# Constant products on TensorE, masks by halves, maxima by tiles and a later weight load in a kernel of clustered attention and two MLPs

## The reference, cut to what is computed

```python
# q, k, v: (2, 8, 768, 64); centroids: (8, 16, 64)
q_assign = argmax(einsum('bhsd,hcd->bhsc', normed(q), normed(centroids)), axis=-1)
k_assign = argmax(einsum('bhsd,hcd->bhsc', normed(k), normed(centroids)), axis=-1)
mask = q_assign[:, :, :, None] == k_assign[:, :, None, :]
scores = where(mask, scale * q @ k.T, -1e9)
attn = exp(scores - max(scores)); attn = attn / (sum(attn) + 1e-9)
x = (attn @ v) as (1536, 512)
# twice: h = x @ w_in (512 -> 2048); g = f(h); x = g @ w_out (2048 -> 512)
# first f: relu with a slope per unit; second f: a ratio of a cubic and a square of h
```

## Time and profile before

| what | us |
|---|---|
| median of 3 runs | 801.58 |
| lowest and highest of them | 801.36 and 802.98 |
| profiled execution, its own time | 800.81 |
| its span | 798.9 |
| TensorE busy (matmuls) in it | 783.6 |
| VectorE busy | 556.3 |
| ScalarE busy | 491.0 |
| GpSimd busy | 295.2 |

### The profile page before, as it was taken

One profiled execution on the slowest core, in us unless ns is written; L12 is line 12 of the kernel. 1 busy time (PEld: TensorE's weight loads), 2 busy tenths in 40 slices (PEclk: granted clock), 3 DMA queues, 4 the chain that ended last, 5 costly groups with the idle time before them and its releaser, 6 DMA issues.

```text
span 798.9 us, 13162 instructions
## 1 busy us (share of the span) xinstructions
PE 783.6 (98%) x4345; PEld 740.3 (93%) x4345; DVE 556.3 (70%) x963; ACT 491.0 (61%) x857; POOL 295.2 (37%) x330
## 2 busy tenths in 40 slices
PE   6999999999999999999999999999999999999997
PEld 5988999999999999999999999999988998999896
DVE  5678878878875555444444454478888888888886
ACT  3766777777887111211211144389999999999996
POOL 7777888988983896000000046540000000000000
PEclk9999999999999999999999999999999999999999
DMA  7636474474332332000000035410001001001001
GB/s 195 187 104 140 119 190 129 118 195 128 83 103 74 100 106 80 0 0 0 0 0 0 0 86 152 123 37 1 1 1 39 0 0 39 0 0 39 1 1 39
DMA packets 30310, 52.15 MB, mean 65 GB/s; under 512 B 9181, under 2 KB 11322, under 8 KB 30266
## 3 DMA queue, kind: packets, MB, share of 16 engines
q1 hardware_dynamic: 30266, 51.59, 23.3%
HBM read 29.40 MB, written 3.19 MB: 41 GB/s over the span
## 4 chain that ended last, share of the span: by engine, by line
PE 83%; DVE 8%; ACT 6%; issue 1%; SPq 1%; DMA 1%; ACTq 0%; DVEq 0%
PE ps L207 28%; PE ps L1193 16%; PE ps L1204 12%; PE ps L724 4%; PE ps L757 4%; PE ps L770 4%; PE ps L809 4%; PE ps L801 4%; PE ps L802 4%; PE ps L694 2%; DVE g_f L1355 1%; ACT scratch L1271 1%; DVE corr L1342 1%; DVE scratch L1351 1%; ACT scratch L1269 1%
## 5 line engine op out<-in xcount | busy, mean ns | idle before, releaser
L213 ACT ACTIVATE g_hi<-g_f 128x384 fp32r<-128x384 f32 x128 | 67.3, 526 | 215.7 <-PE ps L1193 192.5
L217 DVE TENSOR_TENSOR g_lo<-g_f,g_hi 128x384 fp32r<-128x384 f32 x128 | 78.8, 615 | 82.9 <-ACT g_hi L213 82.9
L207 PE MATMUL ps<-x_hi,w_hi_b 128*128 (+1 forms) x352 | 118.8, 337 | 0.0
L207 PE MATMUL ps<-x_hi,w_lo_b 128*128 (+1 forms) x352 | 118.7, 337 | 0.0
L207 PE MATMUL ps<-x_lo,w_hi_b 128*128 (+1 forms) x352 | 118.7, 337 | 0.0
L930 ACT ACTIVATE probs_hi<-ps 128x768 fp32r<-128x768 f32 x96 | 78.1, 813 | 52.7 <-PE ps L770 52.0
L1048 DVE TENSOR_REDUCE row_max<-ps 128x1 fp32r<-128x768 f32 x96 | 90.8, 948 | 23.7 <-PE ps L724 23.6
L391 DVE TENSOR_TENSOR probs_lo<-ps,probs_hi 128x768 fp32r<-128x768 f32 x64 | 60.7, 948 | 15.9 <-ACT ps L933 15.6
L1374 POOL TENSOR_TENSOR w_lo_a<-stage,w_hi_a 128x512 fp32r<-128x512 f32 x10 | 13.3, 1357 | 157.2 <-ACT w_hi_a L1291 157.2
L225 DVE TENSOR_SCALAR corr<-ps,alpha_c 128x384 f32<-128x384 f32 x64 | 39.5, 617 | 45.4 <-PE ps L207 45.0
L391 POOL TENSOR_TENSOR probs_lo<-probs,probs_hi 128x768 fp32r<-128x768 f32 x32 | 58.7, 1835 | 26.7 <-ACT probs L933 26.7
(11 more groups left out here) (132 smaller groups left out, 2086.6 us busy)
## 6 DMA issues: line engine op xcount, KB each, us to landing
stage<-in_moe_w_in SPq DMA_DIRECT2D x27, 256.0 KB, 2.6
stage<-in_moe_w_out SPq DMA_DIRECT2D x27, 256.0 KB, 2.8
raw<-in_qk SPq DMA_DIRECT2D x16, 384.0 KB, 3.8
op_a<-head_hi SPq DMA_DIRECT2D x32, 192.0 KB, 3.3
v_raw<-in_v SPq DMA_DIRECT2D x16, 192.0 KB, 2.5
op_b<-head_hi SPq DMA_DIRECT2D x16, 192.0 KB, 3.3
op_b<-head_lo SPq DMA_DIRECT2D x16, 192.0 KB, 3.5
scratch<-spread SPq DMA_DIRECT2D x16, 192.0 KB, 4.2
```

Of the source, the lines that this page charges most:

```text
L207: last = pe.matmul(h_ps[j % H_RING][:, 0:BLK], a[:, 0, w], x[:, kt, cols], start=(kt == 0 and i == 0), stop=(kt == KT - 1 and i == 2))
L213: act.activation(g_hi[:, j % 2], g_f[:, j % 2], ACT.Copy).then_inc(g_hi_made, 1)
L217: dve.tensor_tensor(g_lo[:, j % 2], g_f[:, j % 2], g_hi[:, j % 2].bitcast(F32), ALU.subtract)\
```

## The change

Nine edits, all in the attention part, most of them before the third head.

1. VectorE first fills 128x256 words of `probs` with 1.0 (read as bf16: 512 columns of zeros and ones). `keep_busy(times)` multiplies this block by itself into PSUM bank 3, which nothing reads: 9 times before the centroids are turned, 2 before `sim(0)`, 4 before `turn_onehot(0)`, 2 behind it, and 1 ahead of each of the first two `turn_first_max`.
2. `sim(1)` stands whole ahead of `turn_onehot(0)` instead of in two parts around it.
3. For heads 0 and 1 `onehot` is made in one VectorE step (`mark_nearest_once`) instead of two.
4. VectorE does `nearest_value(1)` (the maximum) while it waits for `turn_onehot(0)`, and `nearest_equal(1)` behind the q mask, ahead of the first row maximum. Before, both stood behind four row maxima.
5. Head 0's masks release TensorE by halves: the first guard product waits for the first halves alone, its second for all of k, `guard(0, 3)` for all of q.
6. For heads 0 to 3 the turned table is bf16, with both halves beside each other in the same 32 partitions, and written with `transpose`; ScalarE copies each mask of heads 1 to 3 with one instruction of 32x768 instead of two of 32x384.
7. Head 0's first maxima go to `op_b` tile by tile, three ScalarE copies of 1x128; `score_a(0)` stands between the second and the third turn.
8. The written-out order: `weigh_hi(0)`, `turn_onehot(1)`, `score(2)`, `guard(0, 5)` instead of `turn_onehot(1)`, `weigh_hi(0)`, `guard(0, 5)`, `score(2)`; GpSimd does `make_lo(0)` between the high and the low parts of head 2. `copy_first` issues three of head 0's copies as soon as the high parts are there.
9. `load_w` of heads 2 and later moves from the end of iteration `n` of SP's loop to iteration `n + 1`, behind `move_sums(n)`.

The diff, cut to its core:

```diff
+            busy = probs[:, 0, 0:256].bitcast(BF16)
...
             def masks(m, a, r, rows_=32):
-                return ps[a * 64 + r * 32:a * 64 + r * 32 + rows_, 7 if m in (1, 3) else 4, 0:HS]
+                if m < TURNED_BF16:
+                    return masks_bf16(m, r, rows_)[:, a * HS:(a + 1) * HS]
+                return ps[a * 64 + r * 32:a * 64 + r * 32 + rows_, 4, 0:HS]
+
+            def masks_bf16(m, r, rows_=32):
+                return ps[r * 32:r * 32 + rows_, 7 if m in (1, 3) else 4, 0:HS].bitcast(BF16)
+
+            TURNED_BF16 = 4
...
+            def mark_nearest_once(eng, m):
+                eng.wait_ge(onehot_step, 3 * m + 3)
+                at_least(eng, onehot_turned, m)
+                eng.tensor_tensor(onehot[:, :, :, 0:C], first_rank[:].unsqueeze(3).to_broadcast(CLUSTERS), ranks,
+                                  ALU.is_equal).then_inc(onehot_made, 1)
...
+                def copy_first():
...
+                    sp.wait_ge(head_hi_made, 2)
+                    sp.dma_start(bits(qa[0:64]), bits(hi[0:64])).then_inc(a_copied[0], 16)
+                    sp.dma_start(bits(ka[0:64]), bits(hi[64:128])).then_inc(a_copied[0], 16)
+                    sp.dma_start(bits(ka[96:128]), bits(hi[96:128])).then_inc(a_copied[0], 16)
+                    sp.wait_ge(head_split, 1)
+                    sp.dma_start(bits(qa[96:128]), bits(lo[32:64])).then_inc(a_copied[0], 16)
...
                     move_sums(n - 1)
+                    if n - 1 in W_AT[2:] and W_AT.index(n - 1) + 2 < len(W_AT):
+                        load_w(W_AT.index(n - 1) + 2)
...
-                    if n in W_AT and W_AT.index(n) + 2 < len(W_AT):
-                        load_w(W_AT.index(n) + 2)
...
-                split_head(2)
+                split_hi(2, 0)
+                split_hi(2, 1)
                 make_lo(pool, 0)
+                split_lo(2, 0)
+                split_lo(2, 1)
                 split_head(3)
...
+                        if m < TURNED_BF16:
+                            last = pe.transpose(masks(m, t // TH, 0, 64)[:, cols], ones, ident_b[:])
...
-                        pe.wait_ge(mask_q_put, m + 1)
-                        pe.wait_ge(mask_k_put, m + 1)
+                        pe.wait_ge(*((mask_q_put, m + 1) if m else (first_mask_q_put, 1)))
+                        pe.wait_ge(*((mask_k_put, m + 1) if m else (first_mask_k_put, 1)))
+                    if m == 0 and t == FIRST_T:
+                        pe.wait_ge(mask_q_put, 1)
...
                     for a in range(2):
+                        if m == 0 and t == 0 and a == 1:
+                            pe.wait_ge(mask_k_put, 1)
...
+                    at_least(pe, first_max_put, t)
...
+                def keep_busy(times):
+                    for _ in range(times):
+                        pe.matmul(ps[:, 3], busy[:, 0:P], busy, start=True, stop=True)
+
                 pe.sem_inc(h_taken, H_RING)
+                pe.wait_ge(busy_set, 1)
+                keep_busy(9)
...
+                keep_busy(2)
                 pe.wait_ge(cent_put, 2)
                 sim(0)
-                sim(1, range(0, 4))
+                sim(1)
                 pe.wait_ge(ident_made, 4)
+                keep_busy(4)
                 turn_onehot(0)
-                sim(1, range(4, T))
+                keep_busy(2)
                 guard(0, 0)
                 guard(0, 1)
                 guard(0, 2)
+                keep_busy(1)
                 turn_first_max(0)
                 guard(0, 3)
+                keep_busy(1)
                 turn_first_max(1)
+                score_a(0)
                 turn_first_max(2)
-                score(0)
+                score_b(0)
                 guard(0, 4)
                 score(1)
+                weigh_hi(0)
                 turn_onehot(1)
-                weigh_hi(0)
+                score(2)
                 guard(0, 5)
-                score(2)
...
+                for t in range(FIRST_T):
+                    act.wait_ge(first_max_made, t + 1)
+                    act.activation(op_b[96:97, 0, Q_SIDE, t * P:(t + 1) * P], first_max(t, t + 1), ACT.Copy, scale=-1.0)\
+                       .then_inc(first_max_put, 1)
```

74 lines of the change are left out of this document (47 added, 27 removed).

## The result

| kernel | median us | lowest and highest | profiled execution: own time, span |
|---|---|---|---|
| before, on the chip of this comparison | 801.15 (6 runs) | 800.65 to 802.98 | 800.81, 798.9 |
| changed | 796.20 (6 runs) | 795.85 to 796.81 | 796.15, 794.2 |

The ratio is 0.9938, with a 95% interval of 0.9927 to 0.9948: faster by 0.6%. The prediction was 797.0 in a range of 795.6 to 800.4, by a gain of 4.4 us in the profiled execution; the two spans differ by 4.7. The 0.6 us that it added for the median was not there: the changed kernel's median lies 0.05 above its profiled execution. So the forecast holds. Its sum does not hold in the same way: two of its terms are wrong by well over one microsecond each, in opposite directions, and the profile after shows that before any experiment.

What follows compares the result with a forecast made beforehand. TensorE, busy for 98% of the span, bounds the kernel except at the start. 3.75 + 0.35 + 0.3 + 0.3 = 4.7 us, less 0.3 for the clock, gains 4.4: 796.4, plus 0.6 for the median, 797.0 us; range 795.6 to 800.4.

Steps and rivals of the forecast that it cites:

- The clock: At the start, dense wide constant products from about 1.2 us raise TensorE's clock; 0.3 us subtracted for a later rise.
- (a): sim(0) on TensorE, with the clock up, takes 1.26 us instead of 2.78: 1.5 saved.
- (b): One VectorE table step for two, taken at 0.37 us, possibly 0.53: 0.55 saved, 0.37 at worst.
- (c): The turned table on TensorE takes 0.36 us instead of 0.55: 0.2 saved.
- (d): Head 0's masks by halves: first row maximum at 11.2 us instead of 14.07, 2.9 saved so far.
- (f): Last turn, one-tile copy and score_b alone: first scores at 15.3 us instead of 19.05, 3.75 saved in all.
- From the first scores to head 1's guard: Lead grows to 4.1 us, ScalarE ending last, then 0.3 from head 1's masks: first guard at 20.2 instead of 24.61.
- The moved load: Weight load moved in SP's queue: taken as 0, bounds a gain of 0.5 us and a loss of 1.1.
- GpSimd's margin: make_lo(2) leads by only 2.5 us, but weigh_lo on TensorE barely need not wait; a miss costs 0.5 to 1.5.
- The first rival: Clock rises late or falls again between 9.4 and 12.2 us: gain 1.7 to 3.3, time 798.1 to 799.9; chance 0.22.
- The slower rival: Constant products raise nothing and make the turned table 2.1 us late: 803.3 us; chance 0.06.
- That it doesn't do what it says: Clock rises mid sim(1), four constant products end late by what the table gained: about 801.5 us; chance 0.08.

Runs made afterwards that it cites:

- e6: Changed kernel with one ScalarE copy of 384 columns for head 0's three turned maxima instead of three tile copies: 797.05 us, ratio 0.9938.
- e5: Changed kernel with the tables of heads 0 and 1 made in two VectorE steps again: 796.65 us, ratio 0.9935.
- e7: Changed kernel without the eight constant products behind sim(1), the first eleven kept: 798.58 us, ratio 0.9958.
- e9: Changed kernel with GpSimd filling four rows of op_b ahead of split_lo(1)'s subtractions instead of behind them: 796.94 us, ratio 0.9946.
- e4: Kernel before with the memset and the 19 constant products at the same places, nothing else: 802.04 us, ratio 0.9995.
- e8: Changed kernel with all tables turned by plain matmuls with f32 results and mask copies of heads 1 and later in halves: 796.37 us, ratio 0.9937.
- e1: Kernel before with only the load_w of heads 2 and later moved behind the next iteration's move_sums: 799.66 us, ratio 0.9965.
- e2: Changed kernel with only the moved weight load put back at its old place: 801.18 us, ratio 0.9985.
- e11: e2 with both halves of weights 7 loaded ahead of SP's wait for the last reciprocals: 798.54 us, ratio 0.9946.
- e10: Changed kernel with both halves of weights 7 loaded ahead of SP's wait for the last reciprocals: 796.02 us, ratio 0.9918.
- e12: Changed kernel with e10's loads, e9's earlier fill of op_b, and plain matmuls for the tables of heads 0 to 2: 796.32 us, ratio 0.9916.
- e3: Changed kernel without any constant product, the memset kept: 800.40 us, ratio 0.9977.

## Why the prediction was right, point by point

**The clock**: right. Nine wide products raised it, at 3.9 to 5.3 us in the traces of kernels that begin alike (the weight loads of the constant products fall to 0.10 each at 4.05 in e6; the pair of the centroids' turn reads 0.30 at 4.60 in e5 and 0.57 at 4.77 in the changed kernel). The allowance of 0.3 was the right size: the later rise costs 0.35 at `sim(0)`. The profile's granted clock does not show this level, as the prediction said; e7 adds that it does show the level after a fall, as 0.50.

**(a)** `sim(0)` ended at 7.56 instead of 8.71: 1.15 saved; 1.5 less the allowance, right. **(b)** 0.55 expected, hardly 0.2 seen from the end of `sim(0)` to the turned table: the table step took 0.66 and the row before it 0.47. The step that failed is the choice of 0.37, and of 0.53 as the worst: before, both rows stood beside GpSimd's memsets (from 9.64 on), and the new one, at 9.25, stands beside its subtractions (7.72 to 9.68), since the chain came earlier on VectorE and GpSimd's work hardly did. e9 shows it. The reason given for the 0.53, the strided output, was wrong too: the same row takes 0.21 for head 1, in the kernel before at 19.77, with GpSimd idle, so the 0.53 was itself a row slowed by a memset. The Trainium skill has the rule, in "SBUF — State Buffer", Who interferes with whom: an instruction of VectorE with two inputs in SBUF contends with one of GpSimd that reads SBUF, not with one that only writes it. Our rows agree on both halves: 0.65 beside a subtraction, 0.36 beside a memset, and the reduction between them (L1112, one input) stays at 0.35 beside either. **(c)** Nothing saved instead of 0.2. The rule of the Trainium skill on transposes ("TensorE: Matmul & The Clock Gate", Part 4), which the prediction had set against the change, holds as to the rate: at the high clock six transposes take 0.52, six plain products 0.36 (e4, e8). That part of the Trainium skill also says that the high clock does not engage for them, and there the measurement differs and decides: they take 0.82 at the low level (e7) and 0.52 at the high one. And they did not bring the low clock back: e8 and the changed kernel have the same level up to the first scores.

**(d)**, **(e)**: from the masks to the first maximum 1.40 instead of 1.5, three maxima 2.65 instead of 2.8; right, started late. **(f)** is 0.55 too short: 1.86 from the end of the third maximum (14.57) to 16.43, not 1.3. The prediction had one turn, one copy of 0.27, `score_b`, and 0.3 for the chain that copies and turns make. In the trace the third turn starts 0.6 behind the maximum, not 0.3: it waits for the second copy (14.77 to 15.04), and that for the second turn, which stood behind a constant product (to 14.67) that is in the diff and belonged into the step. `score_a`, up to 15.13, adds at most 0.1 to that. The rest is short gaps of 0.02 to 0.14 between the pieces. By e6 the tile copies gain hardly anything over one.

**From the first scores to head 1's guard**: 0.65 expected, 0.25 seen. ScalarE was said to end last, then the masks, 0.3 shorter. ScalarE did end its masks at 21.03, as in e8 with four copies; but TensorE came to the guard at 21.74, behind a row maximum (0.35 idle) and a weighing. The masks of head 1 had cover. Those of head 3, the other 0.3, did not, and paid what was expected.

So the start gave 2.9, with head 3's masks 3.1 to 3.3, and not the 4.7 of the sum, or 4.4 with the clock's allowance.

**The moved load**: the term that failed the other way. I looked at the one DMA behind it in the chain, and at bytes, and bounded it by 0.5. The load's own wait was not priced: by the list of SP's waits it was 7.8 us in five pieces from 95 to 250 us. What it costs reaches TensorE through `move_sums` and `take_pv`. By head 15, and for the same start, that is 1.8 us in the profiles of before and e1 and 2.6 in those of e2 and the changed kernel; by medians it is 2.4 (before against e1) and 2.5 (e11 against e10). The step looked only at what now stands behind the load, `put_max(4, 0)`, where e1 does gain 0.2 (from head 4 to 5), inside the prediction's bounds, and not at the issues that no longer stand behind it: twelve by the list given there, eight copies, a load, two spreads and a move, not eleven.

**GpSimd's margin**: right. `make_lo(2)` ran behind head 3's split without idle time, at 24.66, and TensorE never waited for `weigh_lo`. The margin that was really thin is SP's: e12 crosses it with 3.2 us.

**The first rival** is real: e7 is it, at the predicted price (798.58; the rival's smallest gain, 1.7 against the 4.4 that gave 797.0, makes 799.7, not 799.9). e9, where the clock fell for a while with all 19 products, suggests that the changed kernel is not far from it. **The slower rival** needed a clock still low at 7.5 us; e3 has its order of work at the low clock, without the products, and is 1.5 us behind before at the first turned maxima. That this is close to the rival's 1.7 is chance: the rival put the loss at the first table, and in e3 it comes behind the first scores. e3 ends ahead of before all the same, and of its edits the moved load is the one that gains that much alone (e1). **That it doesn't do what it says** describes no kernel here: e4 ends level with before, but with a clock that is up and a gain that is lost later.

So two errors of the sum, 1.1 to 1.3 too much at the start (4.4 against 3.1 to 3.3) and 1.6 too little at the load (the lead's growth from 3.3 at head 6 to 4.9 at head 15), cancel. That they did so is luck: the forecast's figure was right, and only half of its working was.

**A version that beats both?** e10 has the lowest median of all, 796.02 against 796.20, which these runs can't tell apart; its edit takes away a risk at the seam, no time.

## What to carry to other kernels

Where a step is moved past others in a queue, take the wait that it carries from the list of waits, and follow who needs each instruction behind it; a load that waits for a staging buffer can cost through three engines what its bytes never would. When a chain is shifted in time on one engine, ask anew what the engine beside it does at that moment: what GpSimd was doing made the same row of VectorE 0.36 or 0.65 us long. And a raised clock is worth what the next late thing leaves of it: at head 1 the products gave 4.2 us together with the new order and 0.3 without, and what they gave without it by head 6, 1.1, was lost again at the load and at the seam.

## What the runs showed of the hardware

- Rows of 128x192 in bf16 on VectorE with two SBUF inputs (L1107 of the changed kernel and its like): 0.25 to 0.26 alone or beside a memset of GpSimd, 0.46 (at 8.37) to 1.01 (at 25.62, beside `make_lo`) beside its subtractions. One with a single input: 0.21 alone (before, at 19.77), 0.52 and 0.61 beside memsets (before at 10.59, e5), 1.70 beside subtractions (e4). The slowed two-input rows end 0.1 to 0.2 us behind the GpSimd instruction that ran when they started, the single-input ones 0.06 to 0.07: they wait for its end.
- Six transposes of 128x64 with a bf16 result: 0.52 at the high clock, 0.82 at the low (e7); as plain products with an f32 result 0.36 (e8) and 0.55 (before). Reading two halves of the results, VectorE took 1.01 for bf16 and 1.14 for f32 (e8).
- The granted clock reads 1.00 before the first rise, at durations of the low level (a pair of weight loads 0.57 at 4.77), and 0.50 after a fall (e7).
- After a wait of 1.91 us in full work the clock fell (0.66 of 5 us granted, e6); after the 2.51 us in e4 it did not (products of 384 columns at 0.34 from 21.24 on), nor after the 1.13 at its seam. What decides is not settled here.
- The same DMA of 3 KB landed in 2.0 to 2.1 us in eleven executions and in 3.2 to 3.5 in three. At a place without reserve such a microsecond became 3.6 (e6), with reserve nothing (e11).
